# Spectral filter and two feed-forward stages on one core: the eight filter transfers issued from ScalarE's queue instead of SyncE's

## Chip, cores and metric

The kernel runs on 1 core of one Trainium2 chip. The metric is the device time of one execution in microseconds (us), as the median of three runs.

## What is computed

Three stages follow each other on 6,016 tokens of 256 features. Cut to what matters:

```python
X = np.fft.rfft(x, axis=1)                  # x: (2, 3008, 256)
Y = X * (filt_r + 1j * filt_i)[None]        # 1505 frequencies x 256
y = np.fft.irfft(Y, n=3008, axis=1)
xn = y / sqrt(mean(y * y) + 1e-6) * rms_g   # y as 6016 x 256
h = silu(xn @ w_gate) * (xn @ w_val)        # 256 -> 1536
z = h @ w_out                               # 1536 -> 256
r = maximum(z @ w_in2, 0)                   # 256 -> 2048
out = (s * r * r + b) @ w_out2              # 2048 -> 256
```

## The kernel before, in words

The Fourier transform of length 3008 = 47 x 64 is made of small matrix products. The work of this front stage is cut into 16 chunks q (2 batches times CHUNKS = 8 groups of features). For each chunk:

- SyncE loads x[q] into one of XRING = 3 places of x_ring (load_x, L242: 96 rows of 4 KB, 384 KB). From q = 3 on, that waits until step 1 of chunk q - 3 has read the place.
- TensorE does step 1 in two halves (step1, L328, 8 matmuls against the first part of the tables), ScalarE evicts each half to u_ring (u_out, L521), TensorE does step 2 (L339, against the second part of the tables).
- VectorE multiplies with the filter of this chunk (products, L726 to L728), GpSimd adds the two products (total, L905), TensorE does step 3 (step3, L349), and ScalarE evicts to w_fft (w_out_copy, L527).

There are only 8 filter tiles, f_0 to f_7 (128 rows of 6 KB, 768 KB each): chunk q uses f_tiles[q % 8], so all are loaded once, for the first batch, and stay. Before a filter tile can be used, GpSimd multiplies one half of it by a sign table (sign, L898). In GpSimd's program sign(0) and sign(1) stand ahead of the first total, then sign(q + 2) follows the totals of chunk q.

All transfers of the kernel are issued by SyncE, in one queue, in the order of its program: x[0], the 60 KB part of the tables, x[1], filter 0, the 192 KB part of the tables, filter 1, then x[q] and filter q in turn up to 7, and so on. The order on each engine is written out by hand; engines meet only through semaphores. TensorE begins with two warm-up products on a constant (L320), then step 1 of chunks 0 and 1, step 2 of both, step 1 of chunk 2, and from there a fixed pattern of step 2, step 3, step 1, step 3 for each chunk:

```python
            pe.wait_ge(tab1_in, 16)
            pe.wait_ge(pad_set, 1)
            for q in range(2):
                step1(q, 0)
                step1(q, 1)
            pe.wait_ge(tab2_in, 16)
            step2(0)
            step2(1)
            step1(2, 0)
            step1(2, 1)
            step3(0, 0)
```

When the first batch is through (w_done at 16), SyncE stores w_fft[0] to by_j in HBM in two transfers (L249), loads it back turned (load_z, L253), and TensorE does step 4 (step4, L360), which gives y. Sixteen tiles of 376 tokens then go through the two feed-forward stages (gate_val, down, hidden, project; each product as three matmuls of split operands, L375 to L377). These take most of the time, with TensorE busy throughout.

Of the kernel before, what the change touches and what calls it, by code (L numbers as in the profile page):

```python
# [34 lines left out]
CHUNKS = DIM // (HALVES * 2 * PAIRS)  # L35
# [60 lines left out]
def build(nc, by_j, x, filt, tab, small, w_gate, w_val, w_out, w_in2, w_out2, out):  # L96
    with ExitStack() as ctx:
        def at(name, shape, dt, offset):
            return nc.alloc_sbuf_tensor_at(name, shape, dt, offset=offset)

        def sem(name):
            return ctx.enter_context(nc.semaphore(name))
# [6 lines left out]
        f_tiles = [at(f"f_{n}", [P, 2, 2 * COLS], F32, off) for n, off in enumerate(  # L109
            [OFF_Y + (3 + 6 * n) * KB for n in range(3)] + [OFF_Y + 24 * KB + (3 + 6 * n) * KB for n in range(3)]  # L110
            + [OFF_IN2 + (24 + 6 * n) * KB for n in range(2)])]
# [57 lines left out]
        f_in = [sem(f"f_in{n}") for n in range(CHUNKS)]  # L169
# [38 lines left out]
        def first_pairs(eng, body):  # L208

            body(0, 0, False)  # L210
            body(1, 1, False)
            with eng.Fori(2, TILES - 3, 2) as i:
                body(i, 0, False)
                body(i + 1, 1, False)
            body(TILES - 2, 0, False)
            body(TILES - 1, 1, True)
# [7 lines left out]
        def met(eng):  # L224

            eng.wait_ge(ones_done, 1)
# [9 lines left out]
        @block.sync  # L236
        def _(sp):
            def load_x(q):

                if q >= XRING:  # L240
                    sp.wait_ge(s1_mm, 2 * (q - XRING) + 2)
                sp.dma_start(x_ring[0:XROWS, q % XRING].rearrange("p i c -> p (i c)"), x[q]).then_inc(x_in[q % XRING], 16)  # L242

            def load_f(n):
                sp.dma_start(f_tiles[n][:].rearrange("p k c -> p (k c)"), filt[n]).then_inc(f_in[n], 16)

            def store_w(b, n):
                part = slice(n * NJ // 2, (n + 1) * NJ // 2)
                sp.dma_start(by_j[b, part].rearrange("j p d -> p j d"), w_fft[b][:, part]).then_inc(w_stored[b], 16)  # L249

            def load_z(b, r0, par):
                for rp in range(2):
                    sp.dma_start(z_ring[rp * 48:(rp + 1) * 48, par],  # L253
                                 by_j[b].rearrange("j (c r) d -> (j c) r d", c=2)[:, bass.ds(r0 + rp * R4, R4)]
                                 ).then_inc(z_in[par], 16)

            load_x(0)
            sp.dma_start(tabs[:, 0:TB2], tab[:, 0:TB2]).then_inc(tab1_in, 16)
            load_x(1)
            load_f(0)  # L260
            sp.dma_start(tabs[:, TB2:], tab[:, TB2:]).then_inc(tab2_in, 16)
            load_f(1)
            for q in range(2, 8):
                load_x(q)
                load_f(q)
            load_x(8)
            load_x(9)
            sp.dma_start(consts[:], small).then_inc(consts_in, 16)
            sp.dma_start(gate_raw[:].rearrange("p h f -> p (h f)"), w_gate).then_inc(gate_in, 16)
            load_x(10)  # L270
            load_x(11)
            sp.wait_ge(w_done, 2 * CHUNKS)
            store_w(0, 0)
            load_x(12)
            store_w(0, 1)
            load_x(13)
            sp.wait_ge(w_stored[0], 32)
            load_z(0, 0, 0)
            load_z(0, 8, 1)
            load_x(14)  # L280
            sp.dma_start(val_raw[:].rearrange("p h f -> p (h f)"), w_val).then_inc(val_in, 16)
            load_x(15)
            sp.dma_start(down_raw[:], w_out).then_inc(w1d_in, 16)
            for t in range(2, 4):
                sp.wait_ge(s4_mm, 2 * t - 2)
                load_z(0, 8 * t, t % 2)
            sp.wait_ge(w_done, 4 * CHUNKS)
            for n in range(2):
                store_w(1, n)
            sp.wait_ge(w_stored[1], 32)  # L290
            sp.wait_ge(p_done, 6 * ALL)
            sp.dma_start(in2_raw[:], w_in2).then_inc(in2_in, 16)
            for b in range(BATCH):
                first = b * TILES // 2
                with sp.Fori(4 if b == 0 else first, first + TILES // 2 - 1, 2) as i:
                    for par in range(2):
                        sp.wait_ge(s4_mm, 2 * (i + par) - 2)
                        load_z(b, (i + par - first) * 8, par)

            sp.wait_ge(s4_mm, 2 * TILES)  # L300
            sp.dma_start(out2_raw[:], w_out2).then_inc(out2_in, 16)

            def store(t, par, last):
                met(sp)
                for half, evicted in enumerate((st_act, st_dve)):
                    sp.wait_ge(evicted, t + 1)
                    sp.dma_start(out[bass.ds(t, 1), half].rearrange("t p c -> p (t c)"),
                                 staged[:, par, half]).then_inc(stored[par], 16)

            first_pairs(sp, store)  # L310
            for s in stored:
                sp.wait_ge(s, 16 * HALVES * (TILES // 2))
# [200 lines left out]

        @block.scalar
        def _(a):
            def u_out(q, g):

                a.wait_ge(s1_mm, 2 * q + g + 1)
                if q >= 2:
                    a.wait_ge(s2_mm, q - 1)  # L520
                nc.scalar.copy(u_ring[:, q % 2, g].rearrange("p i c j -> p (i c j)"), bank[g][:, 0:COLS]).then_inc(u_done, 1)  # L521
# [55 lines left out]
            for q in range(3):  # L577
                u_out(q, 0)
                u_out(q, 1)
            w_out_copy(0, 0)  # L580
            w_out_copy(0, 1)
            w_out_copy(1, 0)
            u_out(3, 0)
            u_out(3, 1)
            w_out_copy(1, 1)
# [429 lines left out]
```

## Time and profile before

| | us |
|---|---|
| median of 3 runs | 1262.51 |
| lowest and highest run | 1260.37 and 1262.64 |
| the profiled execution: its own time | 1262.98 |
| the profiled execution: span | 1261.2 |
| TensorE busy in the span | 1244.6 (99%) |
| mean granted clock of TensorE, as a share of full | 0.995 |

The span is the time from the first to the last instruction that the profile shows; the execution's own time lies 1.8 us above it. Engines are named as in the profile: PE is TensorE (PEld its weight loads), DVE VectorE, ACT ScalarE, POOL GpSimd, SPq the instructions that SyncE gives to its DMA queue. "L242" is line 242 of the kernel. A row of the timeline reads: start in us, length in us, engine and line, what it does, how many, and in brackets how long the engine had been idle before and what ended that. In the chain of waits each row is a piece of the chain that ended last.

### The profile page before, as it was taken

To read this page: it belongs to the slowest core of one execution; us is meant where nothing else is said; L and a number is where in the kernel's file an instruction comes from. 1 tells how busy PE (TensorE), PEld (TensorE's weight loads), DVE (VectorE), ACT (ScalarE), POOL (GpSimd) and SP (SyncE) were. 2 spreads that over 40 slices of the span, in tenths; PEclk is the share of its full clock that TensorE was granted. 3 is DMA by queue.
4 is the path that set the end of the run, shared out by engine and by line. 5 is a ranking of instruction groups with operands and counts; after the bars stand their busy time and mean duration, and the time that the engine had idled before them with its cause. 6 is when DMAs were issued, how large, how long until landed. Compare 5 with 4: busy or idle time off the path is not lost.

```text
span 1261.2 us, 20467 instructions
## 1 busy us (share of the span) xinstructions
PE 1244.6 (99%) x7268; PEld 1214.6 (96%) x7268; DVE 683.6 (54%) x1162; ACT 552.3 (44%) x1108; POOL 163.0 (13%) x165
## 2 busy tenths in 40 slices
PE   8979999999999999999999999999999999999998
PEld 5658999999999999999999999999999999999998
DVE  5674454544545445554454375555555555555555
ACT  3444333333333333333344364555454545554554
POOL 7653111011110111101120030000000000000000
PEclk9988999999999999999999999999999999999999
DMA  9855000000000000000010000000000000000000
GB/s 273 246 180 179 14 13 14 1 13 12 13 12 0 12 12 12 12 1 12 0 67 1 2 1 14 13 14 12 12 12 12 12 12 12 12 12 12 13 6 20
DMA packets 16999, 41.07 MB, mean 33 GB/s; under 512 B 1856, under 2 KB 12224, under 8 KB 16320
## 3 DMA queue, kind: packets, MB, share of 16 engines
q1 hardware_dynamic: 16960, 40.55, 10.2%
q8 instruction: 24, 0.39, 0.1%
q14 instruction: 15, 0.12, 0.0%
HBM read 28.10 MB, written 12.45 MB: 32 GB/s over the span
## 4 chain that ended last, share of the span: by engine, by line
PE 96%; DMA 2%; POOL 1%; issue 1%; SPq 0%; DVE 0%; ACT 0%; POOLq 0%; ACTq 0%
PE bank L375 30%; PE bank L376 30%; PE bank L377 30%; PE bank L360 2%; PE bank L328 1%; PE bank L349 1%; DMA by_j<-w_b 1%; PE bank L339 1%; DMA x_ring<-x 1%; POOL spec L905 0%; DMA z_ring<-by_j 0%; PE bank L372 0%; PE bank L371 0%; SPq L242 0%; POOL val_lo L910 0%
## 5 line engine op out<-in xcount | busy, mean ns | idle before, releaser
L773 DVE TENSOR_TENSOR h<-bank,act 128x376 f32<-128x376 f32 x192 | 104.6, 545 | 307.3 <-PE bank L377 298.1
L819 DVE SCALAR_TENSOR_TENSOR h<-act,consts 128x376 f32<-128x376 f32 x256 | 159.7, 624 | 189.4 <-ACT act L637 185.4
L550 ACT ACTIVATE act<-bank 128x376 f32<-128x376 f32 x192 | 93.1, 485 | 369.5 <-PE bank L377 369.3
L637 ACT ACTIVATE act<-bank 128x376 f32<-128x376 f32 x256 | 124.1, 485 | 223.6 <-PE bank L377 223.5
L376 PE MATMUL bank<-h_lo,out_hi 128*128 128x376 f32 x512 | 171.3, 335 | 0.0
L377 PE MATMUL bank<-h_hi,out_lo 128*128 128x376 f32 x512 | 171.3, 335 | 0.0
L375 PE MATMUL bank<-xn_hi,in_hi 128*128 128x376 f32 x512 | 171.1, 334 | 0.2 <-issue 0.2
L375 PE MATMUL bank<-h_hi,out_hi 128*128 128x376 f32 x512 | 171.2, 334 | 0.0
L376 PE MATMUL bank<-xn_lo,in_hi 128*128 128x376 f32 x512 | 171.0, 334 | 0.0
L377 PE MATMUL bank<-xn_hi,in_lo 128*128 128x376 f32 x512 | 170.3, 333 | 0.0
L825 DVE SCALAR_TENSOR_TENSOR h_lo<-h,consts,h_hi 128x376 fp32r<-128x376 f32 x256 | 157.8, 616 | 0.2 <-ACT h_hi L646 0.2
L646 ACT ACTIVATE h_hi<-h,consts 128x376 fp32r<-128x376 f32 x256 | 154.5, 603 | 1.9 <-DVE h L819 1.9
L375 PE MATMUL bank<-xn_hi,gate_hi 128*128 128x376 f32 x384 | 131.6, 343 | 2.9 <-POOL val_lo L910 2.9
L375 PE MATMUL bank<-h_hi,down_hi 128*128 128x376 f32 x384 | 128.4, 334 | 2.6 <-DVE down_lo L740 2.6
L376 PE MATMUL bank<-xn_lo,val_hi 128*128 128x376 f32 x384 | 129.2, 336 | 0.0
L377 PE MATMUL bank<-h_hi,down_lo 128*128 128x376 f32 x384 | 128.9, 336 | 0.0
L376 PE MATMUL bank<-xn_lo,gate_hi 128*128 128x376 f32 x384 | 128.8, 336 | 0.0
L377 PE MATMUL bank<-xn_hi,gate_lo 128*128 128x376 f32 x384 | 128.7, 335 | 0.0
L375 PE MATMUL bank<-xn_hi,val_hi 128*128 128x376 f32 x384 | 128.7, 335 | 0.0
L376 PE MATMUL bank<-h_lo,down_hi 128*128 128x376 f32 x384 | 128.6, 335 | 0.0
L377 PE MATMUL bank<-xn_hi,val_lo 128*128 128x376 f32 x384 | 128.4, 334 | 0.0
L781 DVE TENSOR_TENSOR h_lo<-h,h_hi 128x376 fp32r<-128x376 f32 x192 | 114.1, 594 | 1.1 <-ACT h_hi L559 0.9
(81 smaller groups left out, 2048.2 us busy)
## 6 DMA issues: line engine op xcount, KB each, us to landing
x_ring<-x SPq DMA_DIRECT2D x16, 384.0 KB, 9.5
f<-filt SPq DMA_DIRECT2D x8, 768.0 KB, 12.2
by_j<-w_b SPq DMA_DIRECT2D x4, 1536.0 KB, 8.8
z_ring<-by_j SPq DMA_DIRECT2D x32, 192.0 KB, 2.9
out<-staged SPq DMA_DIRECT2D x32, 188.0 KB, 1.9
in_raw<-w_in SPq DMA_DIRECT2D x1, 2048.0 KB, 7.6
out_raw<-w_out SPq DMA_DIRECT2D x1, 2048.0 KB, 7.6
gate_raw<-w_gate SPq DMA_DIRECT2D x1, 1536.0 KB, 9.7
```

What stands on the lines that cost most here:

```text
L328: mm = nc.tensor.matmul(bank[g][:, i * XROWS:(i + 1) * XROWS], x_ring[:, q % XRING, g * GP + i], tabs[:, 0:TB1], start=True, stop=True)
L360: mm = nc.tensor.matmul(bank[7][:, k * BM:(k + 1) * BM], z_ring[:, par, k, half * P:(half + 1) * P], s4m, start=True, stop=True)
L375: nc.tensor.matmul(acc, hi, xh, start=first, stop=False)
L376: nc.tensor.matmul(acc, hi, xl, start=False, stop=False)
L377: return nc.tensor.matmul(acc, lo, xh, start=False, stop=final)
L550: nc.scalar.activation(act[:, c % 2], bank[2 * (c % 2)][:, 0:TILE], ACT.Silu).then_inc(silu_done, 1)
L637: nc.scalar.activation(act[:, c % 2], bank[c % 4][:, 0:TILE], ACT.Relu).then_inc(relu_done, 1)
L646: nc.scalar.activation(h_hi[:, c % 4], h[:, c % 2], ACT.Identity, bias=bi2).then_inc(gh_done, 1)
L773: nc.vector.tensor_tensor(h[:, c % 2], bank[2 * (c % 2) + 1][:, 0:TILE], act[:, c % 2], ALU.mult).then_inc(hmul_done, 1)
L781: nc.vector.tensor_tensor(h_lo[:, c % 4], h[:, c % 2], h_hi[:, c % 4].bitcast(F32), ALU.subtract).then_inc(hl_done, 1)
L819: nc.vector.scalar_tensor_tensor(out=h[:, c % 2], in0=act[:, c % 2], scalar=sc2, in1=act[:, c % 2], op0=ALU.mult, op1=ALU.mult).then_inc(q ...
L825: nc.vector.scalar_tensor_tensor(out=h_lo[:, c % 4], in0=h[:, c % 2], scalar=bi2, in1=h_hi[:, c % 4].bitcast(F32), op0=ALU.add, op1=ALU.su ...
```

## The change

SyncE no longer issues the filter transfers. ScalarE issues all eight, one after the other and without a wait, as the first instructions of its program, in its own queue. The transfers themselves, their tiles and their semaphores are the same, and so is what waits for them.

```diff
--- before.py
+++ after.py
@@ -241,9 +241,6 @@
                     sp.wait_ge(s1_mm, 2 * (q - XRING) + 2)
                 sp.dma_start(x_ring[0:XROWS, q % XRING].rearrange("p i c -> p (i c)"), x[q]).then_inc(x_in[q % XRING], 16)
 
-            def load_f(n):
-                sp.dma_start(f_tiles[n][:].rearrange("p k c -> p (k c)"), filt[n]).then_inc(f_in[n], 16)
-
             def store_w(b, n):
                 part = slice(n * NJ // 2, (n + 1) * NJ // 2)
                 sp.dma_start(by_j[b, part].rearrange("j p d -> p j d"), w_fft[b][:, part]).then_inc(w_stored[b], 16)
@@ -257,14 +254,9 @@
             load_x(0)
             sp.dma_start(tabs[:, 0:TB2], tab[:, 0:TB2]).then_inc(tab1_in, 16)
             load_x(1)
-            load_f(0)
             sp.dma_start(tabs[:, TB2:], tab[:, TB2:]).then_inc(tab2_in, 16)
-            load_f(1)
-            for q in range(2, 8):
+            for q in range(2, 10):
                 load_x(q)
-                load_f(q)
-            load_x(8)
-            load_x(9)
             sp.dma_start(consts[:], small).then_inc(consts_in, 16)
             sp.dma_start(gate_raw[:].rearrange("p h f -> p (h f)"), w_gate).then_inc(gate_in, 16)
             load_x(10)
@@ -513,6 +505,9 @@
 
         @block.scalar
         def _(a):
+            for n in range(CHUNKS):
+                a.dma_start(f_tiles[n][:].rearrange("p k c -> p (k c)"), filt[n]).then_inc(f_in[n], 16)
+
             def u_out(q, g):
 
                 a.wait_ge(s1_mm, 2 * q + g + 1)
```

On ScalarE, at the start of its program, this stood before (L521 is u_out, L527 is w_out_copy; s1_mm counts the halves of step 1):

```order
L521 ACT_TABLE_LOAD
L521 COPY u_ring_85<-bank0 128x384 [waits s1_mm]
L521 COPY u_ring_85<-bank1 128x384 [waits s1_mm]
L521 COPY u_ring_85<-bank0 128x384 [waits s1_mm]
L521 COPY u_ring_85<-bank1 128x384 [waits s1_mm]
L521 COPY u_ring_85<-bank0 128x384 [waits s2_mm,s1_mm]
L521 COPY u_ring_85<-bank1 128x384 [waits s2_mm,s1_mm]
L527 COPY w_b0_59<-bank6 128x48x8 [waits s3_mm] x3
```

The table load and the eviction of chunk 0 were the first things that ScalarE did. And this stands there now (L509 is the new loop, L516 and L522 are the same two functions):

```order
L509 DMA f_0_50<-filt 128x1536
L509 DMA f_1_51<-filt 128x1536
L509 DMA f_2_52<-filt 128x1536
L509 DMA f_3_53<-filt 128x1536
L509 DMA f_4_54<-filt 128x1536
L509 DMA f_5_55<-filt 128x1536
L509 DMA f_6_56<-filt 128x1536
L509 DMA f_7_57<-filt 128x1536
L516 ACT_TABLE_LOAD
L516 COPY u_ring_85<-bank0 128x384 [waits s1_mm]
L516 COPY u_ring_85<-bank1 128x384 [waits s1_mm]
L516 COPY u_ring_85<-bank0 128x384 [waits s1_mm]
```

Eight DMA instructions stand ahead of the first eviction, and the load of the activation table, which was the first instruction, now comes behind them. On SyncE, at the start of its program, this stood before (L245 is load_f):

```order
L242 DMA x_ring_78<-x 96x1024
L258 DMA tabs_58<-tab 128x120
L242 DMA x_ring_78<-x 96x1024
L245 DMA f_0_50<-filt 128x1536
L261 DMA tabs_58<-tab 128x384
L245 DMA f_1_51<-filt 128x1536
L242 DMA x_ring_78<-x 96x1024
L245 DMA f_2_52<-filt 128x1536
L242 DMA x_ring_78<-x 96x1024 [waits s1_mm]
L245 DMA f_3_53<-filt 128x1536
L242 DMA x_ring_78<-x 96x1024 [waits s1_mm]
L245 DMA f_4_54<-filt 128x1536
```

Each filter stood between two other transfers. And this stands there now:

```order
L242 DMA x_ring_78<-x 96x1024
L255 DMA tabs_58<-tab 128x120
L242 DMA x_ring_78<-x 96x1024
L257 DMA tabs_58<-tab 128x384
L242 DMA x_ring_78<-x 96x1024
L242 DMA x_ring_78<-x 96x1024 [waits s1_mm] x7
L260 DMA consts_93<-small 128x100
L261 DMA gate_raw_64<-w_gate 128x3072
L242 DMA x_ring_78<-x 96x1024 [waits s1_mm] x2
```

The filters are gone from between the x transfers. The first five transfers of SyncE carry no wait in either kernel; the sixth, x[3], waits for step 1 of chunk 0.

## Rows read from the trace of the kernel before

**Rows 1.** The page: busy time of the engines, and the chain by engine.

```profile
PE 1244.6 (99%) x7268; PEld 1214.6 (96%) x7268; DVE 683.6 (54%) x1162; ACT 552.3 (44%) x1108; POOL 163.0 (13%) x165
...
PE 96%; DMA 2%; POOL 1%; issue 1%; SPq 0%; DVE 0%; ACT 0%; POOLq 0%; ACTq 0%
```

**Rows 2.** Chain of waits, 0 to 150 us: start, length, what.

```profile
3.56 10.08 DMA x_ring<-x
13.68 2.02 PE bank L328 x16
...
20.25 1.76 PE bank L328 x16
...
39.31 1.76 PE bank L328 x16
...
53.44 10.97 DMA by_j<-w_b
...
64.78 3.61 DMA z_ring<-by_j
...
70.30 3.25 PE bank L328 x16
```

**Rows 3.** Who waited for whom, 0 to 14 us: total, times, longest.

```profile
POOL f L898 <- DMA f<-filt: 6.1, 2, 4.8
...
PE bank L328 <- DMA x_ring<-x: 1.6, 1, 1.6
```

**Rows 4.** SyncE queue in order of time: start, length, line, transfer.

```profile
2.14 0.43 SPq L245 DMA_DIRECT2D f<-filt  x1
...
3.56 0.43 SPq L242 DMA_DIRECT2D x_ring<-x  x1
4.03 1.37 SPq L245 DMA_DIRECT2D f<-filt  x1
```

**Rows 5.** Transfers issued at 3.56, at 4.03, and the 60 KB table: us to landing.

```profile
x_ring<-x SPq DMA_DIRECT2D x1, 384.0 KB, 10.1
...
f<-filt SPq DMA_DIRECT2D x1, 768.0 KB, 12.1
...
tabs<-tab SPq DMA_DIRECT2D x1, 60.0 KB, 4.1
```

**Rows 6.** DMA, 5 to 40 us: packets and queues.

```profile
DMA packets 2342, 9.86 MB, mean 282 GB/s; under 512 B 409, under 2 KB 537, under 8 KB 2326
...
q1 hardware_dynamic: 2341, 9.84, 99.2%
```

**Rows 7.** GpSimd in order of time: start, length, [idle before <- releaser].

```profile
11.95 1.81 POOL L898 TENSOR_TENSOR f<-f,tabs 128x768 f32<-128x768 f32 x1 [1.31 <-DMA f<-filt]
13.71 1.95 POOL L905 TENSOR_TENSOR spec<-prod 128x384 f32<-128x384 f32 x2
16.17 1.81 POOL L898 TENSOR_TENSOR f<-f,tabs 128x768 f32<-128x768 f32 x1 [0.51 <-DMA f<-filt]
...
20.40 1.81 POOL L898 TENSOR_TENSOR f<-f,tabs 128x768 f32<-128x768 f32 x1 [0.50 <-DMA f<-filt]
```

**Rows 8.** ScalarE in order of time, first instructions.

```profile
0.75 1.28 ACT L521 ACT_TABLE_LOAD   x1 [0.75 <-PEq L1004]
6.54 0.48 ACT L521 COPY u_ring<-bank 128x384 f32<-128x384 f32 x1 [4.51 <-PE bank L328]
```

**Rows 9.** Stretches: length, engines, PEclk, DMA share, GB/s.

```profile
66.90:70.30 3.40, 1.94 (x14) 1.54 (x13) 2.31 (x5) 0.01 (x1) 2.92 (x4) 1.00 0.95 268
70.30:73.70 3.40, 3.40 (x17) 3.40 (x17) 1.49 (x3) 1.07 (x3) 1.00 (x1) 0.50 1.00 349
```

**Rows 10.** TensorE in order of time: first tiles, and step 4.

```profile
5.32 3.86 PE L328 MATMUL bank<-tabs,x_ring 128*128 128x96 f32 x32
9.23 2.85 PE L339 MATMUL bank<-u_ring,tabs 64*128 64x384 f32 x16
...
68.52 1.10 PE L360 MATMUL bank<-consts,z_ring 96*128 96x96 f32 x8 [1.46 <-DMA z_ring<-by_j]
```

## The prediction

> **What bounds the kernel now.** I read the page first, for the engine that sets the end: TensorE is busy 99% of the span and is 96% of the chain that ended last [rows 1]. Work of the other engines costs time only where TensorE waits for it, and the change moves no work on TensorE. So the question is where the filter transfers, or what they share the DMA engines with, hold TensorE up.
>
> The chain of waits answers for the front [rows 2]. Its first long piece is the transfer of x[2], landed at 13.6 us; step 1 of chunk 2 starts at 13.68. The next steps 1 begin at 20.25 (chunk 3) and 39.31 (chunk 7), which is (39.31 - 20.25) / 4 = 4.77 us per chunk, all of it TensorE. The table of who waited for whom shows the same from TensorE's side: it stood 1.6 us for x[2], and GpSimd 6.1 us in two waits for filters 0 and 1 [rows 3]. Until about 64 us no DMA ends a wait of TensorE again; then the store of by_j (53.44, 10.97 us) and the loads of z_ring follow, with 1.46 us of idle time before step 4 [rows 2, 10]. Between them everything hangs on when chunk 2 started: each x[q] is issued when a place of the ring is free, the store when the last w_out_copy of the first batch is done. **A shift of chunk 2 is therefore a shift of the end.**
>
> The DMA engines have no slack there. From 5 to 40 us the one data queue fills 99.2% of 16 engines' time at 282 GB/s [rows 6], and one x and one filter together take 20.40 - 16.17 = 4.2 us by the starts of GpSimd's sign on filters 2 and 3 [rows 7], against TensorE's 4.77 us per chunk. What a filter takes alone: x[2] was issued at 3.56 and landed 10.1 us later, at 13.7; filter 2, directly behind it, was issued at 4.03 and landed 12.1 us later, at 16.1 [rows 4, 5]. That is 2.5 us for 768 KB; the x of a pair is then 4.2 - 2.5 = 1.7 us.
>
> **What the change does.** It removes eight issues from SyncE's queue, of 0.43 us each [rows 4]. Only two of them stand ahead of x[2], so SyncE issues x[2] some 0.9 us earlier, at 2.6. That is worth nothing by itself: x[2] landed 10 us after its issue, because it stood behind other bytes. What counts is which bytes go first. Before, these were x[0], x[1], both tables and **two filters**. Now SyncE's queue holds only the first four, but ScalarE's queue offers all eight filters from about 0.8 us on, and the same engines serve both.
>
> How two queues share the engines, this trace cannot show: all its data went through one queue [rows 6]. The bounds: no filter goes ahead of x[2], which then lands 2 x 2.5 = 5.0 us earlier, at 8.7; or all eight do, 6 x 2.5 = 15.0 us later, at 28.7. I take turns, row against row, since a row is what the profile counts as a packet, and fair turns between two full queues are nearest to neither being preferred. A transfer of 96 rows gives each of the 16 engines 6 rows, one of 128 rows gives 8. Up to x[2], SyncE's queue has 6 + 8 + 6 + 8 + 6 = 34 rows on each engine. In as many turns ScalarE's queue moves 34 / 8 = 4.25 filters. The small rows of the tables (480 bytes and 1.5 KB) each pay for a 6 KB row of a filter. So x[2] waits for 4.25 filters in place of 2: **2.25 x 2.5 = 5.6 us later**, at 19.3.
>
> [...]
>
> Does the rest keep up? Under the same turns, the small table (landed at 1.2 + 4.1 = 5.3 us [rows 5]) has 14 rows and so 1.75 filters with it: +4.4, at 9.7, and step 1 of chunk 0, which began at 5.32 [rows 10], begins then. The second table, with which step 2 began at 9.23 [rows 10], has 28 rows and 3.5 filters with it in place of one: 9.2 + 6.2 = 15.4, and the two steps 2 take 2.85 us, to 18.3. That is ahead of x[2] at 19.3. Filter 1 lands near 10.6 instead of 11.9. After x[2], x[3] needs 1.7 us and 6 / 8 of a filter, 3.6 in all, so it is there at 22.9; it is wanted 20.25 - 13.68 = 6.6 us after chunk 2, at 25.9. Later filters come earlier relative to the chunks than now. So nothing else becomes late, but nothing wins the 5.6 us back either: chunk after chunk takes TensorE its 4.77 us.
>
> ScalarE pays for the issues. Eight at 0.43 and small gaps, 0.47 each, end at 0.75 + 3.8 = 4.5 us. One issue in the trace took 1.37 instead of 0.43: the eighth of SyncE's queue [rows 4]. I add that 0.9 for ScalarE's eighth: 5.5. The table load, 1.28 us, was hidden before and now stands behind them: 6.8 [rows 8]. The first eviction was at 6.54; it is now wanted at 9.7 + 1.2 = 10.9. **Cost nothing, under cover of the later table**; without that cover it would be 0.3 us.
>
> The last term is TensorE's clock. [...] I take 1.0.
>
> Sum: 5.6 + 1.0 = 6.6 us. On the profiled execution's 1262.98 that makes 1269.6; the median of the runs is 0.5 lower, so **1269.1 us**.
>
> **Rivals.**
>
> A. The turns go by bytes, or SyncE's queue is preferred, and nothing measurable changes. By bytes, 1404 KB of SyncE's go with 1404 / 768 = 1.8 filters in place of 2, and x[2] is there at about 13.2; with preference it is earlier. But then filter 1 is late next. It lands when both filters and all five of SyncE's transfers are through, at 13.6 or so instead of 11.9, and sign(1) stands ahead of the first total on GpSimd [rows 7]: 13.6 + 1.8 + 1.0 = 16.4 for the first half of spec. Step 3 of chunk 0, right behind step 1 of chunk 2 (13.68 + 2.0 = 15.7), waits 0.7 to 0.9 us for it. 1262.5 + 0.8 = 1263.3. For it: only that nothing in the trace excludes it. [...]
>
> B. Faster: two queues feed the engines better. The trace reaches 349 GB/s in one stretch against 282 in the front [rows 6, 9]. With order A and that rate TensorE's 1.6 us of idle time goes [rows 3]; with the turns of my forecast, 4.7 MB at that rate still put x[2] near 15.5. 1262.5 - 1.8 = 1260.7, within 0.2%; to be faster by more, the small table would have to land earlier too.
>
> C. ScalarE is held at its last issues until filters have landed. In the SyncE row it was 0.9 us; it decides once the hold lasts beyond about 13 us, since then evictions of chunk 0, and behind them step 1 of chunk 1 and both steps 2, come later than x[2]. Held until filter 3 has landed (near 15.5), the first eviction is at 16.8, steps 1 and 2 end near 22, and chunk 2 starts 2.7 us later than forecast: 1272.
>
> D. All eight filters go first: +15.0, or 1277.5.
>
> **How the numbers follow.** Turns without a hold: 0.58. C: 0.15. D: 0.03. A: 0.19. B: 0.05. A measurement of this kernel can tell about 0.2% (2.5 us) from no change. The forecast, C and D lie beyond it on the slow side: slower 0.76. A and most of B lie within: same 0.20. Faster 0.04. The predicted time is that of the likeliest case. The range runs from 1262, which takes in most of A, to 1274, which takes in C with the clock's 3.0 for my 1.0; half of B, D and some of A stay outside. The likeliest case alone spans 1267.5 to 1271.
>
> **What would show it.** In the new profile, to landing: x[2] about 16.7 us after its issue, the small table 8.5 instead of 4.1; step 1 of chunk 0 near 9.7, of chunk 2 near 19.3, the step from chunk to chunk still 4.77; f 0 and f 1 on GpSimd no longer late. If x[2] lands near 13, A was right; if ScalarE's last filter issue lasts many us, C; if chunk 2 starts late but the end does not, the claim that nothing later takes up the shift is wrong.

## The result, and the profile after

| | before | with the change |
|---|---|---|
| median of 15 runs | 1262.51 us | 1266.18 us |
| lowest and highest | 1259.84 and 1265.24 | 1265.21 and 1270.82 |
| ratio, 95% interval | | 1.0035 (1.0026 to 1.0045) |
| profiled execution, its span | 1261.2 us | 1263.4 us |

The kernel is slower by 0.35%, which is 4.4 us by the ratio and 3.7 by the medians. The page after, answering to [rows 1], hardly moves:

```profile
PE 1245.2 (99%) x7268; PEld 1214.4 (96%) x7268; DVE 684.1 (54%) x1162; ACT 552.4 (44%) x1108; POOL 163.6 (13%) x165
...
q1 hardware_dynamic: 15808, 34.26, 8.5%
q10 hardware_dynamic: 1152, 6.29, 1.5%
...
PE 95%; DMA 2%; POOL 1%; issue 1%; DVE 0%; SPq 0%; ACT 0%; POOLq 0%; ACTq 0%
...
f<-filt ACTq DMA_DIRECT2D x8, 768.0 KB, 16.1
```

TensorE has the same work. The filters now have a queue of their own, q10 (6.29 MB), and take 16.1 us from issue to landing. Its 1152 packets show what a packet is here: 8 filters of 128 rows are 1024, and these alone make up the 6.29 MB; the other 128 are 16 per transfer, as many as there are DMA engines, which I read as its completions. So **a packet is one row or one completion**. q1 has as many fewer than before, 15808 against 16960. What answers to [rows 2] is the chain of waits, 0 to 130 us (start, length, what):

```profile
1.21 8.22 DMA tabs<-tab
9.47 5.84 PE bank L320 x32
15.31 1.51 PE bank L331 x8
...
20.42 1.00 POOL spec L900
21.42 1.77 POOL f L893
23.19 0.96 POOL spec L900
24.19 0.91 PE bank L341 x2
25.11 1.76 PE bank L320 x16
...
39.40 1.76 PE bank L320 x16
...
58.29 10.54 DMA by_j<-w_b
...
72.83 1.10 PE bank L352 x8
```

The first long piece is no longer x[2]. It is the small table, issued at 1.21 and landed at 9.4. Behind it come steps 1 of chunks 0 and 1 (5.84 us, where [rows 10] has 3.86), step 2, the products, and then GpSimd: a total, the sign of filter 2, a total. Step 1 of chunk 3 starts at 25.11, where it was 20.25: **4.9 us later**. From there the chunks are again 4.77 us apart ((39.40 - 25.11) / 3 = 4.76), the store of by_j starts 4.85 us later than in [rows 2] (58.29 against 53.44), and step 4 4.3 us later (72.83 against 68.52 [rows 10]).

TensorE in order of time, 8 to 26 us, shows the same front with its gaps:

```profile
9.47 5.84 PE L320 MATMUL bank<-tabs,x_ring 128*128 128x96 f32 x32 [4.23 <-DMA tabs<-tab]
15.24 2.85 PE L331 MATMUL bank<-u_ring,tabs 64*128 64x384 f32 x16
18.06 2.02 PE L320 MATMUL bank<-tabs,x_ring 128*128 128x96 f32 x16
...
24.19 0.91 PE L341 MATMUL bank<-spec,tabs 128*128 128x384 f32 x2 [1.10 <-POOL spec L900]
24.94 1.92 PE L320 MATMUL bank<-tabs,x_ring 128*128 128x96 f32 x16
```

The gap before the small table is 4.23 us. Step 2 ends at 18.09; x[2], issued at 3.23 us, had landed at 18.0. Both were there at the same moment, so chunk 2 starts at 18.06, 4.4 us later than 13.68. The second table is a third path of the same length: issued at 2.14 us, it took 12.9 us, to 15.0, so step 2 could not have begun much earlier than its 15.24 even with faster steps 1. Chunk 3 follows 24.94 - 18.06 = 6.9 us behind it, of which 1.10 us is a wait for spec.

How the two queues shared the DMA engines: packets of the two queues (a row or a completion each, as the 1152 = 8 x (128 + 16) of q10 show), first from 5 to 9.4 us, then from 9.4 to 13.5 (packets and rate, then for each queue packets, MB, share of 16 engines):

```profile
DMA packets 450, 1.53 MB, mean 347 GB/s; under 512 B 189, under 2 KB 189, under 8 KB 450
...
q10 hardware_dynamic: 226, 1.19, 77.4%
q1 hardware_dynamic: 224, 0.34, 26.2%
...
DMA packets 386, 1.47 MB, mean 357 GB/s; under 512 B 42, under 2 KB 164, under 8 KB 386
...
q10 hardware_dynamic: 196, 1.11, 74.9%
q1 hardware_dynamic: 190, 0.36, 27.6%
```

226 packets against 224, and 196 against 190: the queues take turns by rows, not by bytes, of which there are 1.19 MB against 0.34. Turns of whole transfers would give like counts over several us, so shorter stretches and the landings decide. In four stretches of 0.5 us from 6 us on, the SyncE and ScalarE queues have 34 and 33 packets, 32 and 34, 32 and 30, 29 and 24; whole transfers, in each of which a DMA engine has 8 rows of a filter (an estimate, 128 rows over 16 engines), would show mostly one queue and then mostly the other, unless the 16 engines were out of step. Filter 1 and the small table were both issued at 1.2 us (us to landing):

```profile
f<-filt ACTq DMA_DIRECT2D x1, 768.0 KB, 8.9
tabs<-tab SPq DMA_DIRECT2D x1, 60.0 KB, 8.2
```

They landed at 10.1 and 9.4. Each is the second transfer of its queue; had whole transfers alternated, they would lie one of them apart, 2.5 us for the filter. They lie 0.7 us apart: **one row from each queue in turn**, or at most very few, which these counts do not tell apart.

### The profile page after: what moved, and what is told of

It reads as the page before. It is cut to its first block, busy times and chain, and to the rows that moved or that the text cites. A ratio compares the mean times of both kernels' runs of the same rounds, so it can differ in the third digit from the quotient of the medians.

```text
span 1263.4 us, 20467 instructions
## 1 busy us (share of the span) xinstructions
PE 1245.2 (99%) x7268; PEld 1214.4 (96%) x7268; DVE 684.1 (54%) x1162; ACT 552.4 (44%) x1108; POOL 163.6 (13%) x165
## 3 DMA queue, kind: packets, MB, share of 16 engines
q1 hardware_dynamic: 15808, 34.26, 8.5%
q10 hardware_dynamic: 1152, 6.29, 1.5%
## 4 chain that ended last, share of the span: by engine, by line
PE 95%; DMA 2%; POOL 1%; issue 1%; DVE 0%; SPq 0%; ACT 0%; POOLq 0%; ACTq 0%
PE bank L367 30%; PE bank L368 30%; PE bank L369 30%; PE bank L352 2%; PE bank L320 2%; PE bank L341 1%; DMA by_j<-w_b 1%; PE bank L331 1%; DMA tabs<-tab 1%; POOL spec L900 1%; DMA z_ring<-by_j 0%; PE bank L364 0%; PE bank L363 0%; POOL val_lo L905 0%; POOL gate_lo L905 0%
## 6 DMA issues: line engine op xcount, KB each, us to landing
f<-filt ACTq DMA_DIRECT2D x8, 768.0 KB, 16.1
```

## The experiments

Each was timed beside the kernel before. "Chunk 2" and "chunk 3" are the starts of step 1 of these chunks on TensorE in the profiled execution (13.68 and 20.09 before, 18.06 and 24.94 with the change, whose ratio is 1.0035; the chain of waits cuts pieces a little differently and has 20.25 and 25.11).

| run | median us | ratio to before (95%) | chunk 2 | chunk 3 |
|---|---|---|---|---|
| one queue, order of the turns | 1267.26 | 1.0034 (1.0022 to 1.0047) | 19.41 | 25.82 |
| tiny transfers on ScalarE | 1261.69 | 0.9995 (0.9985 to 1.0005) | 14.22 | 22.27 |
| six filters on ScalarE | 1272.80 | 1.0086 (1.0071 to 1.0101) | 24.41 | 32.47 |
| change, one table | 1267.18 | 1.0041 (1.0028 to 1.0055) | 18.35 | 25.29 |
| change, table load first | 1265.61 | 1.0024 (1.0011 to 1.0037) | 17.01 | 23.93 |
| both | 1265.93 | 1.0024 (1.0011 to 1.0036) | 15.83 | 22.76 |
| two filters first | 1274.28 | 1.0090 (1.0073 to 1.0107) | 17.91 | 24.83 |
| one table, longer warm-up | 1265.84 | 1.0030 (1.0018 to 1.0041) | 17.29 | 24.22 |
| change, three signs first | 1266.77 | 1.0031 (1.0020 to 1.0041) | 18.44 | 25.00 |
| change, no sign between | 1266.45 | 1.0030 (1.0016 to 1.0045) | 19.28 | 25.70 |
| before, one table | 1261.54 | 0.9988 (0.9976 to 1.0000) | 13.72 | 20.13 |
| the same again | 1261.81 | 0.9997 (0.9985 to 1.0008) | 13.59 | 20.00 |

### The order of bytes, or ScalarE's issues?

The theory: what costs is what the DMA engines move ahead of the tables and x[2]. The rival: ScalarE's eight issues and its later table load. Two runs take them apart. The first leaves ScalarE alone and gives SyncE's single queue the order that turns of whole transfers would give:

```diff
             load_x(0)
+            load_f(0)
             sp.dma_start(tabs[:, 0:TB2], tab[:, 0:TB2]).then_inc(tab1_in, 16)
+            load_f(1)
             load_x(1)
-            load_f(0)
+            load_f(2)
             sp.dma_start(tabs[:, TB2:], tab[:, TB2:]).then_inc(tab2_in, 16)
-            load_f(1)
-            for q in range(2, 8):
+            load_f(3)
+            for q in range(2, 6):
                 load_x(q)
-                load_f(q)
+                load_f(q + 2)
+            load_x(6)
+            load_x(7)
             load_x(8)
```

> All transfers back in SyncE's queue, ScalarE issues none, but in the order that turns gave: x[0], filter 0, small table, filter 1, x[1], filter 2, large table, filter 3, x[2], and so on. If the loss is only what goes ahead of the tables and x[2] (theory: turns), the small table lands near 7.7 us, x[2] near 18, chunk 2 starts there (4.4 us later than before) and the time is 1265 to 1267. If the loss comes from ScalarE's own issues and its later table load (rival), it is gone: chunk 2 near 13.7, time 1262.5.

Measured: 1267.26 us, ratio 1.0034: the whole loss, with no DMA instruction on ScalarE. TensorE in order of time:

```profile
6.39 2.02 PE L332 MATMUL bank<-tabs,x_ring 128*128 128x96 f32 x16 [1.20 <-DMA tabs<-tab]
11.38 3.36 PE L332 MATMUL bank<-tabs,x_ring 128*128 128x96 f32 x16 [2.97 <-DMA x_ring<-x]
14.67 4.80 PE L343 MATMUL bank<-u_ring,tabs 64*128 64x384 f32 x16
19.41 2.02 PE L332 MATMUL bank<-tabs,x_ring 128*128 128x96 f32 x16
```

The small table was there at 6.3 already and chunk 0 started then, earlier than expected, but x[1] came behind two more filters, 2.97 us after TensorE wanted it, and then steps 1 and 2 were slow (3.36 and 4.80 us; the granted clock was 0.50 from 12 to 18 us in this execution). x[2], issued at 4.5 us, took 13.6 us, to 18.1, as forecast and as with the change (18.0): the order alone puts it there. But TensorE was busy with step 2 until 19.4, so the loss of the same size came by another link, x[1] and the slow steps behind it.

The second run is the kernel before, with eight tiny transfers as ScalarE's first instructions:

```diff
         def _(a):
+            for n in range(CHUNKS):
+                a.dma_start(spare[16 * n:16 * n + 16], tab[16 * n:16 * n + 16, 0:2]).then_inc(tiny_in, 16)
```

(ScalarE also waits for tiny_in before its first write to spare, in chunk 12.)

> The kernel before, with eight transfers of 16 rows of 8 bytes issued by ScalarE as its first instructions. Theory of turns: ScalarE is busy with issues to about 4.6 us, its table load ends near 5.9, before the first eviction at 6.5; step 1 of chunk 2 stays at 13.7 and the time at 1262.5. Rival, the issues on ScalarE cost the time: chunk 2 near 18, time about 1266.

Measured: 1261.69, ratio 0.9995 (0.9985 to 1.0005), no loss. ScalarE in order of time:

```profile
0.74 3.90 ACTq L518 DMA_DIRECT2D spare<-tab  x8
4.68 1.28 ACT L525 ACT_TABLE_LOAD   x1 [4.68 <-issue]
6.10 0.48 ACT L525 COPY u_ring<-bank 128x384 f32<-128x384 f32 x1
```

Issues to 4.64, table load to 5.96, first eviction at 6.10, ahead of the 6.54 of [rows 8]. (Chunk 3 at 22.27 in the table belongs to this one execution, the slowest of its 12 with 1265.73 us, in which step 1 of chunk 2 took 3.33 us; the ratio rests on all of them.) With the change itself the issues run from 0.74 for 4.75 us and the table load ends at 6.8, where the first eviction is wanted at 11.5. **The rival falls**: ScalarE's issues cost nothing that these runs can tell in either case.

### A larger dose

Filters 0 and 1 back in SyncE's queue, where they stood, and filters 2 to 7 from ScalarE first:

```diff
-            for n in range(CHUNKS):
+            for n in range(2, CHUNKS):
                 a.dma_start(f_tiles[n][:].rearrange("p k c -> p (k c)"), filt[n]).then_inc(f_in[n], 16)
```

> The change, but filters 0 and 1 stay in SyncE's queue where they were; filters 2 to 7 are issued by ScalarE first. Theory of turns: the small table lands near 9.4 as with the change, but SyncE's queue has 50 rows per DMA engine up to x[2] instead of 34, and the 16 more are filter rows that alternate with filter rows: filter 0 lands near 17, x[2] near 27, chunk 2 starts 13 us later than before, time about 1275. Rival, ScalarE's issues: six in place of eight, so a smaller loss than the change, at most 1265.

Measured: 1272.80, ratio 1.0086. Fewer filters on ScalarE, and more than twice the loss. x[2] landed at 24.4 (forecast 27) and chunk 2 started there:

```profile
3.88 20.49 DMA x_ring<-x
...
24.41 3.02 PE bank L325 x16
```

The direction and the order of size are those of the turns: 16 more rows of filters stand in SyncE's queue, each with a filter row of the other queue beside it. The turn was cheaper than assumed, as with the change itself.

### Which transfer governs?

Both tables in one transfer, of 2,016 bytes per row, take 128 rows out of SyncE's queue ahead of x[2], eight per DMA engine if they are spread evenly, and no bytes:

```diff
-            sp.dma_start(tabs[:, 0:TB2], tab[:, 0:TB2]).then_inc(tab1_in, 16)
+            sp.dma_start(tabs[:], tab).then_inc(tab1_in, 16)
             load_x(1)
-            sp.dma_start(tabs[:, TB2:], tab[:, TB2:]).then_inc(tab2_in, 16)
```

(Step 2 then waits for tab1_in in place of tab2_in.)

> The change, but both tables are loaded by one transfer of 128 rows of 2,016 bytes in the place of the small one, which takes 8 rows per DMA engine (9 turns with the completion) out of SyncE's queue ahead of x[2]. Theory of turns: x[2] lands 9 turns of 0.31 us = 2.8 us earlier, near 15.3; if turns went by bytes it would stay near 18. If x[2] alone set the start of chunk 2, that start moves to 15.4 and the time to 1263.5; if the landing of the first table (9.4) and TensorE's work on chunks 0 and 1 behind it (8.6 us) set it just as well, chunk 2 stays near 18 and the time near 1266.

Measured: x[2], issued at 2.1, took 13.3 us and landed at 15.5, 2.5 us earlier than with the change. So a short row costs about a whole turn: by estimate 2.5 / 9 = 0.28 us for each of 8 rows and a completion, where a row of a filter took 2.5 / 8 = 0.31. And yet chunk 2 started at 18.35 and the time was 1267.18, no better. The transfer of x[2] and the chain of waits:

```profile
x_ring<-x SPq DMA_DIRECT2D x1, 384.0 KB, 13.3
...
1.21 8.17 DMA tabs<-tab
...
9.42 6.22 PE bank L319 x32
15.64 1.51 PE bank L330 x8
```

So **x[2] did not govern alone**: the first table, landed at 9.4, and the work of TensorE behind it were just as long. A second run says the same from the other side. ScalarE issues only filters 0 and 1 first, the others between its evictions:

```diff
-            for n in range(CHUNKS):
-                a.dma_start(f_tiles[n][:].rearrange("p k c -> p (k c)"), filt[n]).then_inc(f_in[n], 16)
+            load_f(0)
+            load_f(1)
...
             for q in range(3):
                 u_out(q, 0)
                 u_out(q, 1)
+                if q:
+                    load_f(q + 1)
```

and filters 4 to 7 one chunk apart after that (load_f holds the same transfer).

> ScalarE issues only filters 0 and 1 first, filter 2 after its evictions of chunk 1, filter 3 after those of chunk 2, the others one chunk apart. Up to x[2] the DMA engines move the same two filters as in the kernel before, so x[2] lands near 13. Theory, the small table governs: it still takes its turns with filter rows, lands near 9.4, TensorE then needs 8.6 us for chunks 0 and 1, chunk 2 starts near 17 to 18, time 1265 to 1266. Rival, x[2] governs: chunk 2 near 13.7, time 1262.5.

Measured: x[2] landed at 12.8, chunk 2 still started at 17.91: the small table, landed at 9.3, governed. The time, 1274.28, is not a verdict on this, because the later filters, issued one chunk apart, came too late. What GpSimd waited for, 24 to 56 us:

```profile
34.90 1.80 POOL L901 TENSOR_TENSOR f<-f,tabs 128x768 f32<-128x768 f32 x1 [5.56 <-DMA f<-filt]
...
f<-filt ACTq DMA_DIRECT2D x1, 768.0 KB, 7.4
```

The filter issued at 27.5 took 7.4 us, with SyncE's queue moving 0.78 MB, about two x, beside it. My expectation had overlooked that.

### Why the chain behind the small table is long

Three parts: the landing of the table, the slow steps 1, and GpSimd. In the change itself the slow steps are nearly covered by the second table (15.0); with one table they are not.

**The landing.** ScalarE first copies one column of the warm-up tile, so that its table load comes first and its issues start later:

```diff
+            a.wait_ge(warm_set, 1)
+            nc.scalar.copy(spare[:, 0:1], warm[:, 0:1])
             for n in range(CHUNKS):
```

> The change, but ScalarE first does one tiny eviction of the warm-up tile, so its table load comes ahead of its eight issues and filter 0 is issued near 2.3 us instead of 0.75: x[0] and most of the small table are through by then. Theory (the small table's landing starts the chain): the small table lands near 5.9 instead of 9.4, step 1 of chunk 0 starts there, chunk 2 near 14.5 (x[2] lands near 14.3), time 1263 to 1263.5. Rival, what counts is only how many filter rows go ahead of x[2]: x[2] still needs some 27 turns with filters and lands near 16 or later, time 1265.

Measured: issues from 1.45 us on (2.3 expected), the small table at 4.3, chunk 0 at 5.04, as early as ever. x[2] landed at 14.9, near the 14.3 expected, so the rival falls. But the time was 1265.61, not 1263.3:

```profile
5.04 2.06 PE L320 MATMUL bank<-tabs,x_ring 128*128 128x96 f32 x16
9.28 3.73 PE L320 MATMUL bank<-tabs,x_ring 128*128 128x96 f32 x16 [2.18 <-DMA x_ring<-x]
12.94 4.13 PE L331 MATMUL bank<-u_ring,tabs 64*128 64x384 f32 x16
17.01 2.02 PE L320 MATMUL bank<-tabs,x_ring 128*128 128x96 f32 x16
```

Now x[1] was late, by 2.18 us, and steps 1 and 2 behind it took 3.73 and 4.13 us (2.06 before it, and 2.85 in the change), at a granted clock of 0.50 from 9 to 15 us. With one table on top:

> The same, and both tables in one transfer. x[2] loses 9 more turns and lands near 12; chunk 2 starts at 12.5 to 13, time 1261.5, a little under the kernel before. If the table of 128 rows of 2 KB lands late (near 7, behind filter 0), step 1 of chunk 0 waits for it and chunk 2 starts near 14: 1263.

Measured: x[2] landed at 12.5, near the 12 expected, but chunk 2 started at 15.83: x[1] had landed at 9.4, at the end of its own turns, and TensorE needed to 15.8 for chunk 1 and both steps 2. 1265.93, ratio 1.0024. Step 2 took 3.92 us there, where it takes 2.85 with the change, and the granted clock was 0.73 from 12 to 16 us. So two things are left in the median: x[1] still pays for its rows, and the steps behind the gaps are slow. No run separates them. Three of the twelve executions of this version took 1261.8 to 1261.9 us, at a mean granted clock of 0.996 where the profiled one had 0.993; the fastest executions of the kernel before, beside them, took 1260.3 us. Those three come near the 1261.5 expected.

**The slow steps 1.** The change with one table, and six warm-up products instead of two:

> The change with both tables in one transfer, and six warm-up products instead of two, so TensorE has work until near 9 us. If the granted clock is up when step 1 of chunk 0 starts at 9.4, steps 1 of chunks 0 and 1 take 3.9 to 4.9 us (x[1] lands at 12.4) instead of 6.2 and chunk 2 starts near 17.1 instead of 18.5: time 1.4 us under the run with one table alone, near 1265.8. If the clock is not the cause of the 6.2 us, nothing changes.

Measured:

```profile
9.79 1.92 PE L319 MATMUL bank<-tabs,x_ring 128*128 128x96 f32 x16
12.55 2.02 PE L319 MATMUL bank<-tabs,x_ring 128*128 128x96 f32 x16 [0.85 <-DMA x_ring<-x]
14.51 2.85 PE L330 MATMUL bank<-u_ring,tabs 64*128 64x384 f32 x16
17.29 2.02 PE L319 MATMUL bank<-tabs,x_ring 128*128 128x96 f32 x16
```

Steps 1 took 1.92 and 2.02 us instead of 6.22 together, and chunk 2 started at 17.29, forecast 17.1, against 18.35. The warm-up products ran to 9.95 us. With TensorE kept at work through the gap, the same 32 matmuls took 3.94 us (3.86 in the kernel before); with 4.2 us of idle time before them they took 6.22, over half as long again. The median moved from 1267.18 to 1265.84, against 1.4 forecast, though the two intervals overlap.

**GpSimd.** With eight filters first on ScalarE and two signs first on GpSimd, chunk 3 started 6.9 us behind chunk 2 in every run of the table; it was 6.4 before. The sign of filter 2 stands in GpSimd's program between the totals of chunks 0 and 1. The first attempt to move it put all signs one place earlier:

```diff
-            for n in range(2):
+            for n in range(3):
                 sign(n)
...
-                if q + 2 < CHUNKS:
-                    sign(q + 2)
+                if q + 3 < CHUNKS:
+                    sign(q + 3)
```

> The change, but GpSimd signs three filters ahead of its first total instead of two, so no sign stands between the totals of chunks 0 and 1. Filter 2 lands near 13.3, long before. Theory (GpSimd's order sets the start of chunk 3, 9.8 us after the first step 2): chunk 3 loses its wait of 1.1 us for spec and starts 6.6 us after chunk 2, near 24.6, instead of 25.1; the time falls by 0.5, near 1265.7. If that wait is not of GpSimd's order, chunk 3 stays 7.05 us behind chunk 2.

That left a sign in the same place, now that of filter 3. It was my edit that missed its aim, and the wait for spec only fell with chunk 2's own delay (6.56 us, with 0.78 us of waiting left). The second has nothing there (`if 0 < q < CHUNKS - 2: sign(q + 2)`):

> The change, with GpSimd signing filter 2 ahead of its first total and nothing between the totals of chunks 0 and 1 (the run with three signs first still had sign(3) there). Theory (GpSimd's sign between them sets the start of chunk 3): the total of chunk 1 starts at 22.1 instead of 23.2, right after VectorE's products; TensorE no longer waits for it, and chunk 3 starts 6.6 us after chunk 2, near 24.6. The time falls by 0.5 at most, less than a comparison resolves. Otherwise chunk 3 stays 7 us behind chunk 2.

Measured: GpSimd, then TensorE, in order of time:

```profile
23.45 1.00 POOL L900 TENSOR_TENSOR spec<-prod 128x384 f32<-128x384 f32 x1 [0.76 <-DVE prod L723]
...
9.74 6.83 PE L320 MATMUL bank<-tabs,x_ring 128*128 128x96 f32 x32 [4.50 <-DMA tabs<-tab]
...
19.28 2.02 PE L320 MATMUL bank<-tabs,x_ring 128*128 128x96 f32 x16
...
24.98 0.88 PE L341 MATMUL bank<-spec,tabs 128*128 128x384 f32 x2 [0.66 <-ACT w_b L522]
25.70 1.47 PE L320 MATMUL bank<-tabs,x_ring 128*128 128x96 f32 x12
```

The total of chunk 1 follows VectorE's products, and chunk 3 starts 6.42 us behind chunk 2, as before the change; the wait that is left is for ScalarE. (Chunk 2 itself was late in this execution, because steps 1 took 6.83 us, again at a granted clock of 0.50.) The time, 1266.45, is not told apart from the change's.

### Fewer rows in one queue

If small rows cost a turn beside another queue, do they cost anything in a queue of their own? The kernel before, with one table transfer:

> The kernel before with both tables in one transfer, everything in SyncE's queue. SyncE's queue has 8 rows per DMA engine fewer ahead of x[2]: by the small table's 1.3 us between the landings of x[0] and itself, x[2] would land up to 1 us earlier than 13.6, chunk 2 start near 12.8, and the time fall to 1261.7, under both kernels; if small rows cost next to nothing in a queue of their own, nothing changes: 1262.5.

Measured: x[2] landed at 13.7 and chunk 2 started at 13.72, as before. The median was nevertheless 0.12% lower, so it ran once more:

> The kernel before with one table transfer, once more: in the first run its median lay 0.12% under before (interval 0.24% to 0.00% under) while chunk 2 started at 13.72, as before. If the gain is real, the ratio is again near 0.999; if it was scatter, it is 1.000.

Measured: 0.9997 (0.9985 to 1.0008). No gain, and the first is put down to scatter. No version beat the kernel before clearly.

## Why the prediction was right, and where it was not

The direction, the place and the cause were right: 1269.1 us forecast, 1266.18 measured, inside the range of 1262 to 1274. That range says little, since it holds the kernel before (1262.51) as well. The size was not right: +6.6 us against +3.7 to +4.4.

- **Turns, row against row**: right. The queues' packets are 226 and 224, 196 and 190, as shown above. The landings of filter 1 and the small table, 0.7 us apart, speak against turns of whole transfers (2.5 us). That a packet is a row shows in the 1152 of q10. The 6 and 8 rows per engine are an estimate, 96 and 128 rows over 16 engines; no view gives rows by engine.
- **The small table at 9.7, step 1 of chunk 0 there**: right; 9.43 and 9.47.
- **x[2] at 19.3, "2.25 x 2.5 = 5.6 us later"**: the term that was mis-sized. It landed at 18.0, 4.4 us later. The count of rows was about right: from 2 us to the landing of x[2] the engines moved 3.51 MB before and 5.40 MB with the change, 1.89 MB or 2.4 filters more. The rate was not: I had priced a filter at 2.5 us in a front at 282 GB/s, and over these stretches the engines moved 302 GB/s before and 338 with the change.
- **"So nothing else becomes late"**: the step that failed. I had the end of steps 2 at 18.3, which is what came (18.09), but counted it as covered by x[2] at 19.3. With x[2] at 18.0 the margin was gone. The run with one table shows it: x[2] 2.5 us earlier and no gain. The small table, 5.84 us of steps 1 and step 2 reach the same 18.06 as x[2]. And because steps 2 now end when x[2] lands, not 1.6 us ahead, VectorE's products come later relative to chunk 2, and the sign of filter 2, hidden before, delays chunk 3 by another 0.5 us (6.88 against 6.41 us behind chunk 2).
- **ScalarE's issues cost nothing, under cover of the later table**: right. Issues to 5.5 and table load to 6.8 were forecast; they were 5.49 and 6.80. The run with tiny transfers gives the price without cover: none either.
- **The clock, 1.0 us**: no run shows this term, nor the 3.0 that the range allows for it; both were my estimates. What the runs showed in its place: steps 1 of chunks 0 and 1 took 5.84 us after the gap, where they took 3.86 before, 2.0 us more, but under cover of the second table and x[2]. Further on, the profiled execution got some back. TensorE at 0.50 of its clock in stretches of the kernel before and then with the change (length, busy time of PE, PEld, DVE, ACT, POOL, PEclk, DMA share, GB/s):

```profile
90.80:97.60 6.80, 3.86 (x13) 3.78 (x13) 3.75 (x7) 0.96 (x2) 6.68 (x7) 0.50 0.00 0
107.90:111.30 3.40, 3.40 (x13) 3.40 (x12) 1.41 (x2) 0.09 (x1) 2.04 (x3) 0.51 1.04 337
```

```profile
92.30:102.50 10.20, 7.64 (x21) 5.92 (x21) 5.39 (x10) 2.00 (x6) 7.08 (x8) 0.50 0.00 0
```

Before, the stretches at half clock are 3.4 [rows 9], 6.8 and 3.4 us, 13.6 in all; with the change one of 10.2. Within one stretch of 3.4 us, step 1 at 70 us took 3.25 us in place of 1.76 [rows 2, 9], 1.5 us more, so by estimate 3.4 us less is worth about that. That goes most of the way to the 2.2 us by which the spans of the two profiled executions differ, where chunk 3 differs by 4.9 and step 4 by 4.3. The other runs fit: the two runs of the kernel before with one table had 10.2 us of such stretches, chunk 3 where it was, and spans of 1259.7 and 1259.9, 1.3 to 1.5 under 1261.2. Nor are they alone. From the start of chunk 3 to the end of the span, the five profiled executions with 13.6 us at half clock in that part (the kernel before, tiny transfers, one table, load first, both) took 1240.4 to 1241.7 us; of the eight with 10.2 us, seven took 1238.4 to 1239.9 and the run with one queue 1240.8. (The run with two filters first is left out, since its later filters held it up.) No run sets these stretches by itself, so that they account for the remainder is not tested. The profiled execution with the change was also the fastest of its 15 (1265.21 us).
- **"A shift of chunk 2 is a shift of the end"**: mostly. 4.9 us at chunk 3, 4.85 at the store, 4.3 at step 4, since the store took 10.54 us instead of 10.97 and TensorE waited 0.91 us there instead of 1.46. Why is open: the same store took 10.56 to 12.21 us in the other runs, 12.21 and 11.40 in the two of the kernel before with one table.
- Rivals: A fell with the packet counts. B's higher rate was there (338 GB/s against 302), and made the loss smaller, not a gain: by the landing of x[2] 5.40 MB had been moved, not the 4.7 that I had reckoned with for B's 15.5 us. C did not occur; the longest of ScalarE's eight issues took 1.14 us. The 0.9 us that I read from the eighth issue is no rule either: in the run with one queue ten issues in a row took 0.40 to 0.44 us each.

## What to carry to other kernels

A second queue was not a side road here: its rows alternated about one for one with those of the first (226 packets against 224), so bulk that was not needed soon delayed what was: x[2] by 4.4 us, the tables of 128 short rows from 4.1 to 8.2 us (60 KB) and from 6.6 to 12.9 (192 KB) from issue to landing. In a front like this one, what it waits for belongs ahead of the bulk, in one queue whose order says what is urgent; moving the bulk to an engine with free issue time took 0.43 us per issue off SyncE's queue here, and nothing waited for that. And before pricing a shift by one late transfer, follow each of the other first transfers through the work behind it: removing the lateness of x[2] here gained nothing.

## What the runs showed that was not expected

- The engines moved more with the change: from 10 to 25 us 332 GB/s against 274 in the same stretch of the kernel before. The mix of rows differs as well (3.44 MB of 4.99 are filters with the change). The run with one queue, in nearly the same order, had 299 GB/s, so part of the difference comes without a second queue; what the rest is owed to is open.
- With the change the table of stretches gives a granted clock of 1.00 from 9.4 to 15.3 us, but 32 matmuls of step 1 took 5.84 us after 4.2 us of idle time, 3.86 without it, and 3.94 after a longer warm-up. ScalarE's evictions of their four halves began at 11.53, 13.23, 14.46 and 15.35 us: 1.70 us apart at first and 0.89 at the end. In the kernel before they are 0.89 apart throughout; in the run with no sign between, where the column gives 0.50 from 9.5 to 16 us, they are first 1.70 and 1.71 apart. So in this stretch the durations tell more than the column.
- The same instructions of step 1 (16 matmuls) and of both steps 2 in the first three chunks took 1.9 to 3.7 and 2.9 to 4.8 us in the profiled executions of the different versions, and one version's executions lie up to 7 us apart (1261.79 to 1269.05 us for the run called both), so the front of a single execution can be some us off its median.
